# Attention and two gated layers on one core: TensorE's order by shapes of weights, sums in quarters of the columns, EPS on VectorE

## What is computed

```python
factor = 4; Sd = 144
q_d, k_d, v_d = means over 4 tokens                     # coarse attention, 144 x 144
out_up = repeat(softmax(q_d k_d^T / 8) v_d, 4)
mask = abs(pos[:, None] - pos[None, :]) < 4             # local attention, a band of 7 keys
out_local = softmax(where(mask, q k^T / 8, -1e9)) v
x = (out_up + out_local) as 2304 x 512
x = (sigmoid(x @ w_gate) * (x @ w_val)) @ w_out         # 512 -> 1536 -> 512
h = x @ w_in2                                           # 512 -> 2048
out = (h * sigmoid(1.702 h)) @ w_out2                   # -> 512
```

## Time and profile before

| what | us |
|---|---|
| median of three executions | 870.51 (868.97 to 871.15) |
| the profiled execution | 871.78, its span 870.0 |
| PE busy | 857.4 (99%), 6638 matmul records, as many weight loads |
| DVE busy | 621.7 (71%) |
| ACT busy | 487.3 (56%) |
| POOL busy | 590.0 (68%) |
| packets on the queue called "instruction" (q8) | 53, 0.87 MB |

### The profile page before, as it was taken

One profiled execution on the slowest core, in us unless ns is written; L12 is line 12 of the kernel. 1 busy time (PEld: TensorE's weight loads), 2 busy tenths in 40 slices (PEclk: granted clock), 3 DMA queues, 4 the chain that ended last, 5 costly groups with the idle time before them and its releaser, 6 DMA issues.

```text
span 870.0 us, 18366 instructions
## 1 busy us (share of the span) xinstructions
PE 857.4 (99%) x6638; PEld 832.4 (96%) x6638; DVE 621.7 (71%) x1140; ACT 487.3 (56%) x1083; POOL 590.0 (68%) x471
## 2 busy tenths in 40 slices
PE   8999999999999999999999999999999999999998
PEld 6777899999999999999999999999999999999998
DVE  5767645554657685868676877777878778878777
ACT  5778754545536364645354656654676466556652
POOL 6678878988759648885457776763668644856523
PEclk9999999999999999999999999999999999999999
DMA  9877466685956887838588825245246751636432
GB/s 335 259 217 235 144 242 242 228 340 207 384 161 196 293 291 287 301 107 299 198 277 303 288 88 205 99 144 198 67 172 218 267 178 65 218 131 224 168 120 73
DMA packets 74777, 184.26 MB, mean 212 GB/s; under 512 B 5568, under 2 KB 31168, under 8 KB 71872
## 3 DMA queue, kind: packets, MB, share of 16 engines
q1 hardware_dynamic: 74688, 183.10, 60.0%
HBM read 141.66 MB, written 41.42 MB: 210 GB/s over the span
## 4 chain that ended last, share of the span: by engine, by line
PE 93%; issue 2%; DVE 1%; POOL 1%; DMA 1%; ACT 1%; SPq 1%; ACTq 0%; DVEq 0%
PE o_ps L787 10%; PE o_ps L789 10%; PE o_ps L788 10%; PE d_ps L641 7%; PE d_ps L642 7%; PE d_ps L643 7%; PE s_ps L641 6%; PE o_ps L632 6%; PE s_ps L643 6%; PE s_ps L642 6%; PE t_ps L641 3%; PE t_ps L642 3%; PE t_ps L643 3%; PE o_ps L605 2%; PE o_ps L625 1%
## 5 line engine op out<-in xcount | busy, mean ns | idle before, releaser
L787 PE MATMUL o_ps<-g_hi,v 128*128 128x384 f32 x504 | 169.5, 336 | 0.7 <-DVE att L1752 0.6
L789 PE MATMUL o_ps<-g_hi,v 128*128 128x384 f32 x504 | 169.3, 336 | 0.0
L788 PE MATMUL o_ps<-g_lo,v 128*128 128x384 f32 x504 | 169.2, 336 | 0.0
L1752 DVE TENSOR_TENSOR att<-o_ps,att 128x384 f32<-128x384 f32 x212 | 118.1, 558 | 55.9 <-PE o_ps L789 53.4
L2102 POOL TENSOR_TENSOR v<-v_f,v 128x512 fp32r<-128x512 f32 x72 | 95.4, 1346 | 56.2 <-ACT v L1055 56.2
L2102 POOL TENSOR_TENSOR v<-raw,v 128x512 fp32r<-128x512 f32 x54 | 71.0, 1314 | 89.3 <-ACT v L1048 75.9
L641 PE MATMUL d_ps<-xs_hi,w 128*128 128x384 f32 x360 | 120.9, 336 | 2.0 <-issue 1.2
L643 PE MATMUL d_ps<-xs_hi,w 128*128 128x384 f32 x360 | 120.3, 334 | 0.0
L642 PE MATMUL d_ps<-xs_lo,w 128*128 128x384 f32 x360 | 120.3, 334 | 0.0
L641 PE MATMUL s_ps<-xs_hi,w 128*128 128x384 f32 x300 | 101.0, 337 | 1.4 <-POOL xs_lo L2132 1.4
L643 PE MATMUL s_ps<-xs_hi,w 128*128 128x384 f32 x300 | 100.3, 334 | 0.0
(11 more groups left out here) (186 smaller groups left out, 2099.6 us busy)
## 6 DMA issues: line engine op xcount, KB each, us to landing
w<-w_split SPq DMA_DIRECT2D x48, 768.0 KB, 7.0
w<-w_split SPq DMA_DIRECT2D x48, 512.0 KB, 7.9
w<-w_split SPq DMA_DIRECT2D x96, 256.0 KB, 4.9
w_split<-w SPq DMA_DIRECT2D x12, 1792.0 KB, 6.7
raw<-in_w_out_dram SPq DMA_DIRECT2D x36, 512.0 KB, 4.5
w_split<-job_w SPq DMA_DIRECT2D x8, 1792.0 KB, 7.9
vw<-in_v_win_dram SPq DMA_DIRECT2D x16, 390.0 KB, 4.8
raw<-in_w_gate_val_dram SPq DMA_DIRECT2D x12, 512.0 KB, 3.9
```

The source lines that it names most:

```text
L787: pe.matmul(bank, vh, gh, start=(start and k == c), stop=False, skip_group_check=True)
L788: pe.matmul(bank, vh, gl, start=False, stop=False, skip_group_check=True)
L789: mm = pe.matmul(bank, vl, gh, start=False, stop=(k == c + 1), skip_group_check=True)
L1752: vec.tensor_tensor(part, value, part, ALU.add).then_inc(y_added, 1)
```

## The change

1. `masks(u)` runs four matmuls with weights 64x64 in place of two with 64x128, with the same result.
2. `sum_values`, `sum_values_1` and `weigh_pooled` write 32 partitions by each matmul (weights 128x32): each of the five tiles of v has its own 32 rows, and `weigh_pooled` has 8 matmuls for 4. `fours` shrinks to 32 columns.
3. TensorE's loop: `score(i + 2)` stands ahead of `turn(i + 1)`.
4. `turn` begins with the pairs of the second bank and counts `turned` twice; `copy_turned` copies that bank first, and counts `copied` twice. `weigh_pooled` waits for the first of the two.
5. EPS is added by VectorE, just ahead of its reciprocal, on which it then waits for itself; GpSimd's addition and its waits are gone.
6. GpSimd's sums for the second block of weights (`sum_in_1(1)` to `sum_in_4(1)`) move from steps 8 to 11 to steps 3, 4, 6 and 7; `low_x_sum` of T3 moves from step 13 to 14 and of T4 from step 14 behind the loop.
7. SyncE: `load_in(1)` from step 4 to 2, `load_out(0)` from step 1 to 4.

```diff
-                for h in range(2):
-                    rows = slice(h * HK, (h + 1) * HK)
-                    pe.matmul(s_ps[:, h, 0:PAIRS * KW], picks[rows, :], mask[rows, :, :], start=True, stop=False)
+                for par in range(2):
+                    out_rows = slice(par * HK, (par + 1) * HK)
+                    for h in range(2):
+                        rows = slice(h * HK, (h + 1) * HK)
+                        pe.matmul(s_ps[out_rows, h, 0:PAIRS * KW], picks[rows, out_rows], mask[rows, :, :], start=True, stop=False)
...
-                for j in (0, 2, 1, 3, 4):
-                    bank, at = divmod(j // 2 * 64, P)
-                    pe.matmul(d_ps[at:at + 64, bank, VS_AT:VS_AT + P], fours[:, j % 2, :], vt[u % 2][:, j, :],
-                              start=(j % 2 == 0), stop=(j % 2 == 1 or j == VT - 1))
+                for j in range(VT):
+                    bank, at = divmod(j * VK, P)
+                    pe.matmul(d_ps[at:at + VK, bank, VS_AT:VS_AT + P], fours[:, :], vt[u % 2][:, j, :], start=True, stop=True)
...
-                for pair in range(PAIRS):
+                for pair in (*range(PT0, PAIRS), *range(PT0)):
                     mm = pe.transpose(...)
-                mm.then_inc(turned, 1)
+                    if pair in (PT0 - 1, PAIRS - 1):
+                        mm.then_inc(turned, 1)
...
-                    for h in range(2):
-                        rows = slice(h * D, (h + 1) * D)
-                        mm = pe.matmul(t_ps[rows, 1, OD_AT:OD_AT + SD], v_sum[u % 2][:, c, rows], pd_t[:, h, c, :],
+                    for n in range(4):
+                        rows = slice(n * VK, (n + 1) * VK)
+                        mm = pe.matmul(t_ps[rows, 1, OD_AT:OD_AT + SD], v_sum[u % 2][:, c, rows], pd_t[:, n // 2, c, :],
...
                 masks(i + 2)
+                score(i + 2)
                 turn(i + 1)
-                score(i + 2)
...
             def inverse_pooled(u):
+                dve.wait_ge(exped_d, u + 1)
+                vec.tensor_scalar(plus_d[0:HQ, :], den_d[u % 2][0:HQ, :], EPS, None, ALU.add).then_inc(plus_ready_d, 1)
                 dve.wait_ge(plus_ready_d, u + 1)
```

More of the change, by code:

```diff
@@ L35 @@
 VT = 5
+VK = P // FACTOR
 HQ = SD // 2
@@ L197, in attention_mlp_kernel @@
         picks = place("picks", [P, P], BF16)
-        fours = place("fours", [P, 2, P // 2])
+        fours = place("fours", [P, VK])
         warm = place("warm", [P, 2 * P], BF16)
@@ L540, in sum_values @@
                     pe.wait_ge(v_summed, u)
-                for j in (0, 2, 1, 3, 4):
-                    bank, at = divmod(j // 2 * 64, P)
-                    pe.matmul(d_ps[at:at + 64, bank, VS_AT:VS_AT + P], fours[:, j % 2, :], vt[u % 2][:, j, :],
-                              start=(j % 2 == 0), stop=(j % 2 == 1 or j == VT - 1))
+                for j in range(VT):
+                    bank, at = divmod(j * VK, P)
+                    pe.matmul(d_ps[at:at + VK, bank, VS_AT:VS_AT + P], fours[:, :], vt[u % 2][:, j, :], start=True, stop=True)
             def sum_values_1():
                 pe.wait_ge(vt_loaded[1], 16)
[L549 to L552, removed]
+                for j in range(VT):
+                    c, at = divmod(j * VK, P)
+                    mm = pe.matmul(t_ps[at:at + VK, 1, VS1_AT + c * P:VS1_AT + (c + 1) * P], fours[:, :], vt[1][:, j, :],
+                                   start=True, stop=True)
                 mm.then_inc(sums_turned, 1)
@@ L594, in weigh @@
             def weigh(u):
[L596 removed]
+                pe.wait_ge(copied, 2 * u + 2)
                 pe.wait_ge(vw_loaded[u % 2], 16 * (u // 2) + 16)
@@ L961, in copy_turned @@
                     act.wait_ge(weighed, u)
-                for b, pairs in enumerate((range(PT0), range(PT0, PAIRS))):
-                    c = nc.scalar.copy(p_t[:, 2 * pairs.start:2 * pairs.stop, 0:QW],
-                                       t_ps[:, b, 0:len(pairs) * P].rearrange("p (w k) -> p w k", k=HK)[:, :, 0:QW])
-                c.then_inc(copied, 1)
+                for n, (b, pairs) in enumerate(((1, range(PT0, PAIRS)), (0, range(PT0)))):
+                    act.wait_ge(turned, 2 * u + n + 1)
+                    nc.scalar.copy(p_t[:, 2 * pairs.start:2 * pairs.stop, 0:QW],
+                                   t_ps[:, b, 0:len(pairs) * P].rearrange("p (w k) -> p w k", k=HK)[:, :, 0:QW]).then_inc(copied, 1)
             def copy_turned_pooled(u):
@@ L2022, in normalise_pooled @@
             def normalise_pooled(u):
-                pool.wait_ge(exped_d, u + 1)
-                if u >= 1:
-                    pool.wait_ge(inv_ready_d, u)
-                gp.tensor_scalar(plus_d[0:HQ, :], den_d[u % 2][0:HQ, :], EPS, None, ALU.add).then_inc(plus_ready_d, 1)
                 pool.wait_ge(inv_ready_d, u + 1)
```

35 lines of the change are left out of this document (17 added, 18 removed).

## The result

| | before | after |
|---|---|---|
| median of the executions compared (us) | 870.38 (868.97 to 871.15) | 878.15 (874.74 to 880.36) |
| profiled execution, its span | 871.78, 870.0 | 874.74, 872.6 |
| attention loop, 2nd `weigh` to the 15th | 19.42 to 101.93: 82.51 | 19.02 to 104.62: 85.60 |
| behind the loop | 768.08 | 767.98 |

The change makes the kernel slower: the ratio is 1.0078, 95% interval 1.0054 to 1.0102. I had predicted 863.7. Each median is of four executions. The profiled execution of after is the fastest of its four. It shows 3.0 us of the loss, 2.6 in its span and 0.4 outside of it (874.74 less 872.6 against 871.78 less 870.0); the other executions, up to 5.6 us longer, have no trace. Their mean granted clock is 0.998, 0.996 and 0.996, and that of the profiled one 0.996, so what they have more is not time at a low clock.

The account below looks back on a forecast made before the run. TensorE's own queue was taken to bound the attention loop. 13 x (6.045 - 5.47) = 7.5, + 0.35 at the start, - 1.0 for gaps, saves 6.8 us: median 870.51 to 863.7, range 860.4 to 869.0.

Parts of the forecast that it names:

- the order by shapes: TensorE's loop: with equal weight shapes adjacent, three of eight shape changes go, -0.435 us a unit.
- the masks: TensorE's masks in 64x64: two additional matmuls fit the same round, cost 0, at worst +0.14 us a unit.
- the sums: TensorE's sums in quarters: 4 rounds for 6, -0.22 us a unit.
- EPS: Addition moved to VectorE: about 0.2 us more work there a unit, covered, so cost 0.
- the forecast of 5.47 a step: Attention loop: a unit of TensorE falls from 6.045 to 5.47 us.
- the wait for `normed`: Ahead of `turn_out`, TensorE waits for VectorE's result: +0.08 us a unit, bounds 0 and 0.15.
- Rival A: Quarters in the loop run two at a time, not four: 6.07 us a unit, 871 us; chance 0.09.
- +0.24 a unit: Rounds in quarters: by the skill's factor 2.38 they take a quarter more, median about 866.7 us.
- Rival C: ScalarE or GpSimd paces the loop's units: 5.65 us instead of 5.47, 866 us; chance 0.15.
- the start (-0.35): Ahead of the loop: faster sums and one shape change less in the start-up groups, -0.35 us.
- the term for the gaps, +1.0: TensorE's "issue" gaps in the loop: one gap more, +1.0 us, bounds -1.8 and +4.
- rival B: Instruction supply decides the loop: at 5.9 us a packet a unit takes 7.3, 886 us; chance 0.06.

Follow-up runs that it names:

- pooled_halves: The changed kernel with pooled weighing in four matmuls as before, 292 records a step; median 872.36 us, ratio 1.0014.
- old_loads_prep: The changed kernel with the loads and GpSimd's preparation back at their old steps; median 878.38 us, ratio 1.0085.
- before_shifted: The kernel before with 128 more instructions ahead of the loop and the loop itself the same; median 875.50 us, ratio 1.0047.
- before_more_records: The kernel before with each mask matmul cut in six, 308 records a step for 288; median 876.55 us, ratio 1.0067.
- after_light: The changed kernel with loads of v cut to a fifth and a sixth from the third unit on, output incomplete; median 872.53 us, ratio 1.0018.
- old_order: The changed kernel with turn ahead of score in TensorE's loop as before; median 875.77 us, ratio 1.0055.
- half_sums: The changed kernel with masks, pooled weighing and sums as before, 288 records a step; median 873.72 us, ratio 1.0042.
- after_shifted: The changed kernel with 128 more instructions ahead of its loop and none in it; median 876.76 us, ratio 1.0068.
- quarter_sums: The changed kernel with masks and pooled weighing as before, sums still in quarters, 288 records a step; median 875.40 us, ratio 1.0059.
- order_only: The kernel before with only score moved ahead of turn in TensorE's loop, 288 records a step; median 876.21 us, ratio 1.0063.

## Why the prediction was wrong

**Right: the order by shapes, the masks, the sums, EPS (the forecast of 5.47 a step).** It is 5.42, between 5.39 without the wait for `normed` and 5.47 with it. Three changes of shape gone, 0.145 each, were read from single rounds; pooled_halves puts one back for 0.15. Sums in five quarters take 0.52 to the next start for 0.75. The wait came where I put it and cost less than the +0.08: `turn_out` starts 2.30 behind `weigh` (49.11 for 46.81), 0.09 after VectorE's multiply ends, as its timeline in after shows:

```profile
47.79 0.23 DVE L1533 RECIPROCAL small<-o_ps 128x12 f32<-128x12 f32 x1 [0.47 <-PE o_ps L608]
48.06 0.96 DVE L1537 TENSOR_TENSOR o_tok<-o_ps,small 128x768 f32<-128x768 f32 x1
```

Quarters of 32 columns run four at a time: pooled weighing takes 0.52 for 16 records where it took 0.54 for 8. Rival A is out. The Trainium skill's factor of 2.38 for three weights of 32 columns ("TensorE: Matmul & The Clock Gate", section "Why this matters for your kernels"), by which I had estimated +0.24 a unit, is not borne out here: four such weights run at the rate of two of 64 columns. No run shows one of them alone.

**Right: what other engines do.** Rival C did not come. In the loop VectorE ends 0.2 us of PE's waits in all. GpSimd's preparation and the loads are worth nothing that can be seen (old_loads_prep).

**Right: the start (-0.35) and the layers.** -0.40, and 767.98 for 768.08.

**Wrong: the term for the gaps, +1.0, with bounds -1.8 and +4.** It was +6.2, and +3.4 for the clock behind them, which I had not in the sum at all. With the rest of +1.6 this is 11.2, where I had 1.0; 0.4 more lies outside the span. The step that failed is "I take one gap more". I had the break-even in hand (4.9 us a packet; asked for were 4.44), and the row that spoke for it, six packets in 35.5 us. I set against it that four came in 13.5 us. By the starts above, these four are the catching up behind a gap, not a pace to count on. What the runs showed in its place: TensorE stops at every border of 256 instructions whose packet has not landed 1.2 us before. The time between two borders fell from 5.28 to 4.43 us and took the slack with it, from some 3.0 to 2.1 us, while the packets went on starting up to 3.9 us behind the border before. The gaps went from 3 to 10. That one packet comes in each step until TensorE is dry, which with 37 instructions a step over 256 would happen 13 x 37/256 = 1.9 times in the loop and with 57 over 2.9 times, fits the groups of both kernels and most of before_shifted, and is not more than a reading.

**Right in kind, too strong in size: rival B**, to which I gave 0.06. It took 5.9 us as the price of each packet, and 16 us. In truth a loop of 16 packets takes 85.6, 5.4 a packet, as before_more_records has it too (86.04). The slower form of 5.9 holds in stretches.

**Not explained.** What lets a packet start, and why in before six in a row start at nearly one place of the step. It is not the end of one load: the last landing before these starts is of v at 54.71, of k at 59.57, 66.15, 71.69 and 78.09, and of v again at 82.58, 2.2 us ahead of 84.74. Light loads shorten the distance of the starts (52.78, 58.18, 63.58, 69.76, 75.19, 81.06: 5.66 on the mean, for 5.99 in the kernel before), which points to the transfers; but after_light still has gaps of 1.5 and 1.6. Not explained either is why five kernels with the same 293 instructions differ by 5.8 us in their medians (870.4 to 876.2). The phase of the packets may be one part (before_shifted). A large part of the loss of after, 7.8 by the medians and 3.0 by the profiled executions, is in executions that I have not seen inside. No version beats both kernels: the best complete one, pooled_halves, is at 872.36 against 871.16, and level by the span.

## What to carry to other kernels

Count the instructions of the engine that bounds a stage, weight loads and f32 passes and waits too, and set the time of 256 of them against the distance of the packets on its instruction queue. Where "issue" gaps already show, an edit that buys time with more and shorter instructions buys nothing; here 20 more records in each of 13 steps of 6 us cost 0.67%, a part of it ahead of the loop, and 16 fewer gave back 0.64% (1.0078 to 1.0014); but kernels with the same 288 records differ by 0.6%, so the count gives the direction and not the size. To tell this wait from others, count the engine's instructions up to each gap: here all were a multiple of 256 apart. Order and weight shapes are free of that price and worth 0.145 us for each change of shape, but they, too, raise the pace at which instructions are asked for. And a gap's place and size on one trace depend on what stands ahead of the loop: 128 instructions there moved the first long one by 23 us and made it 1.8 times as long.

## What the runs showed of the hardware that I had not expected

- Packets of 16,384 bytes, 256 instructions by the distance of the gaps, each about 1 us long. All 80 gaps "<-issue" of 0.3 us or more in the first 110 us of the 15 traces stand at a border of 256, and TensorE goes on 1.20 to 1.62 us after the packet has landed. A packet starts at most 288 instructions ahead of its use.
- The granted clock fell to 0.50 behind gaps of 2.66 and 2.45 (after), 1.84 and 1.91 (old_order), 2.67 (before_shifted), 2.49 (half_sums), 1.64 (after_light, at 101.70) and even 1.40 (after_shifted, at 64.50), each time for 3.41 us; it was at 0.50 for 6.83 behind 2.19 (old_loads_prep) and, from within the gap on, with 3.36 (after_shifted); with 2.69 (quarter_sums) it fell within the gap too, for 3.41. Behind 2.35 (half_sums), 2.08 and 2.25 (pooled_halves) and 1.80 (order_only) it stayed at 1.00. The length of the gap alone does not tell which it will be.
- Weights 128x32, four side by side, run at the rate of two of 128x64: 16 rounds in 0.52 for 8 in 0.54.
- The place where TensorE waits within a step is not a matter of what stands there but of where the 256th instruction falls: 3.36, 2.83, 2.69, 2.67 and 2.66 us were all inside or at the end of `score`, between matmuls that wait for nothing.
